# Attention and two MLPs in one kernel: groups of turned blocks without empty columns, an earlier request for auxiliary rows, a weight split in 16 pieces, x halves and sums in other places

## What is computed

```python
# 4 batches, 8 heads each (32 heads), 576 positions, head size 64
scores = q @ k.T / 8
cum = cumsum(max(s, 0))
scores = where(causal, -1e9, scores + min(-(cum_i - cum_j), 0))
attn = softmax(scores);  x = attn @ v            # tokens 2304, width 512
h = x @ w_in                                     # 512 -> 1024
solu = h * softmax(h);  x2 = layernorm(solu) * g_ln @ w_out   # 1024 -> 512
out = max(x2 @ w1, x2 @ w2, x2 @ w3) @ w_out2    # 512 -> 768 -> 512
```

## Time and profile before

| | |
|---|---|
| runs | 734.2, 733.35, 732.66 us; median 733.35 |
| the profiled execution | 731.73 us, its span 729.9 us |
| granted TensorE clock | 0.999 of full speed |
| TensorE matmul | 704.8 us busy, 97% of the span |
| VectorE | 388.5 us, 53%; from 100 to 200 us: 95.0 us of 100 |
| ScalarE | 319.0 us, 44%; from 100 to 200 us: 89.3 us of 100 |
| GpSimd | 253.6 us, 35%; from 100 to 200 us: 86.6 us of 100 |
| DMA | 59.5 MB, 82 GB/s over the span; 160 to 220 GB/s in the attention stage |

### The profile page before, as it was taken

One profiled execution on the slowest core, in us unless ns is written; L12 is line 12 of the kernel. 1 busy time (PEld: TensorE's weight loads), 2 busy tenths in 40 slices (PEclk: granted clock), 3 DMA queues, 4 the chain that ended last, 5 costly groups with the idle time before them and its releaser, 6 DMA issues.

```text
span 729.9 us, 12004 instructions
## 1 busy us (share of the span) xinstructions
PE 704.8 (97%) x4032; PEld 621.7 (85%) x4032; DVE 388.5 (53%) x681; ACT 319.0 (44%) x752; POOL 253.6 (35%) x284
## 2 busy tenths in 40 slices
PE   3899999999999999999999999999999999999998
PEld 3798898888887898989898998888888888888897
DVE  7999999999968556363635445510320132022121
ACT  3899998899865335242424423311210121111111
POOL 8767778898889464343101000000000000000000
PEclk9999999999999999999999999999999999999999
DMA  6577777778476140900000031001000000100000
GB/s 185 169 205 228 190 199 190 190 195 227 124 175 145 46 87 11 250 0 1 1 1 1 0 116 58 0 1 58 0 1 30 29 1 1 57 1 0 30 30 30
DMA packets 57721, 59.52 MB, mean 82 GB/s; under 512 B 23060, under 2 KB 44692, under 8 KB 57652
## 3 DMA queue, kind: packets, MB, share of 16 engines
q1 hardware_dynamic: 57684, 59.02, 30.1%
HBM read 44.15 MB, written 10.10 MB: 74 GB/s over the span
## 4 chain that ended last, share of the span: by engine, by line
PE 77%; DVE 9%; issue 6%; ACT 5%; POOL 3%; DVEq 0%; ACTq 0%; POOLq 0%
PE ps L680 10%; PE ps L682 10%; PE ps L681 10%; PE ps L597 5%; PE ps L599 5%; PE ps L598 5%; PE ps L523 4%; PE ps L525 4%; PE ps L524 4%; PE ps L489 4%; PE ps L698 3%; PE ps L700 3%; PE ps L699 3%; DVE q_a L1063 3%; DVE nmax L1070 3%
## 5 line engine op out<-in xcount | busy, mean ns | idle before, releaser
L682 PE MATMUL ps<-x_lo,w_hi 128*128 128x512 f32 (+1 forms) x360 | 132.4, 368 | 0.0
L681 PE MATMUL ps<-x_hi,w_lo 128*128 128x512 f32 (+1 forms) x360 | 132.4, 368 | 0.0
L680 PE MATMUL ps<-x_hi,w_hi 128*128 128x512 f32 (+1 forms) x360 | 132.4, 368 | 0.0
L870 ACT ACTIVATE probs<-ps,nmax 128x576 f32<-128x576 f32 (+4 forms) x160 | 82.9, 538 | 6.7 <-DVE nmax L1070 6.7
L489 PE MATMUL ps<-ident,probs 128*128 128x128 f32 x480 | 75.8, 282 | 8.4 <-DVE pt_lo L1077 5.6
L1077 DVE TENSOR_TENSOR pt_lo<-ps,pt_hi 128x512 fp32r<-128x512 f32 (+1 forms) x128 | 78.3, 653 | 7.7 <-ACT pt_hi L880 4.8
L682 PEld LDWEIGHTS ps<-x_lo,w_hi 128*128 128x128 f32 x360 | 67.9, 189 | 11.3
L681 PEld LDWEIGHTS ps<-x_hi,w_lo 128*128 128x128 f32 x360 | 67.9, 189 | 11.2
L680 PEld LDWEIGHTS ps<-x_hi,w_hi 128*128 128x128 f32 x360 | 67.9, 189 | 11.2
L880 ACT ACTIVATE pt_hi<-ps 128x512 fp32r<-128x512 f32 (+1 forms) x128 | 69.8, 574 | 11.6 <-PE ps L489 9.3
L471 PE MATMUL ps<-k_a,q_a 128*128 128x288 f32 (+2 forms) x192 | 63.2, 336 | 11.4 <-POOL qk_b L743 10.8
(11 more groups left out here) (100 smaller groups left out, 1416.9 us busy)
## 6 DMA issues: line engine op xcount, KB each, us to landing
qk_raw<-in_qk_dram SPq DMA_DIRECT2D x32, 576.0 KB, 4.4
xT<-halves SPq DMA_DIRECT2D x32, 144.0 KB, 2.4
xb_dram<-halves SPq DMA_DIRECT2D x32, 144.0 KB, 2.4
xb<-xb_dram SPq DMA_DIRECT2D x24, 192.0 KB, 3.7
rinvB<-rsum_dram SPq DMA_DIRECT2D x24, 192.0 KB, 4.7
stage<-in_moe_w_dram SPq DMA_DIRECT2D x18, 256.0 KB, 4.6
out_dram<-stage SPq DMA_DIRECT2D x18, 256.0 KB, 2.0
v_raw<-in_v_dram SPq DMA_DIRECT2D x32, 128.0 KB, 3.7
```

The source lines that it names most:

```text
L680: pe.matmul(dst, w_hi[f][:, i, c, :], x2_hi[par][:, c, 0:w], start=(c == 0), stop=False)
L681: pe.matmul(dst, w_lo[f][:, i, c, :], x2_hi[par][:, c, 0:w], start=False, stop=False)
L682: mm = pe.matmul(dst, w_hi[f][:, i, c, :], x2_lo[:, c, CT * g:CT * g + w], start=False, stop=(c == KC - 1))
L870: act.activation(dst, SCORES[c], ACT.Exp, bias=nmax[par][:, c:c + 1], accum_out=sums_all[:, c, bass.ds(t, 1)]).then_inc(exp_done, 1)
```

## The change

It has five parts. The groups of turned blocks are put together anew and the area of `pt_hi` and `pt_lo` is laid out to match, and group 0 leaves out the 64 empty columns of block (0, 0). SP requests the auxiliary rows of head t-1 before it waits for and requests q and k of head t. `w_in` is split in 16 pieces of 256 columns, one after each slot from slot 12 to 27. In the first MLP's group 0 the x halves for the next group come before the exponential on ScalarE, and on VectorE right after the maximum, with `wout_low` in their old place. VectorE inverts the sums of heads 0 to 23 after slot 26.

```diff
-    J2, J0, J1, J4, J3, TW = 0, 3 * P, 8 * P, 12 * P, 13 * P, 15 * P
+    J0, J2, J1, J4, J3, TW = 0, 5 * P, 8 * P, 12 * P, 13 * P, 15 * P
     GROUPS = [
-        ([(2, 2), (2, 3), (2, 4), (0, 0)], J2),
-        ([(0, 1), (0, 2), (0, 3), (0, 4)], J0 + P),
+        ([(0, 0), (0, 1), (0, 2), (0, 3)], J0),
+        ([(0, 4), (2, 2), (2, 3), (2, 4)], J0 + 4 * P),
...
-        WPIECES = 8
+        WPIECES = 16
         WPIECE = KC * FF // WPIECES
+        WFIRST = HEADS // 2 - 2 - WPIECES // 2
...
             def reload(t, par, known=None):
+                if known == 3:
+                    sp.wait_ge(aux_stored, 16)
+                if known is None or known >= 3:
+                    reload_aux(t - 1, 1 - par)
                 sp.wait_ge(k_hi_ready, t - 1)
                 sp.wait_ge(q_lo_ready, t - 1)
                 sp.wait_ge(k_lo_ready, t - 1)
                 load_qk(t, par)
                 if known is None or known >= 4:
                     reload_v(t - 2, par)
-                if known == 3:
-                    sp.wait_ge(aux_stored, 16)
-                if known is None or known >= 3:
-                    reload_aux(t - 1, 1 - par)
...
-            FIRST = HEADS // 2 - 1 - WPIECES
-            with pool.Fori(2, FIRST) as pair:
+            with pool.Fori(2, WFIRST) as pair:
...
-            with pool.Fori(FIRST, HEADS // 2 - 1) as pair:
+            with pool.Fori(WFIRST, WFIRST + WPIECES // 2) as pair:
                 t = 2 * pair
                 slot(t, 0, None)
+                split_win(t - 2 * WFIRST)
                 slot(t + 1, 1, None)
-                split_win(pair - FIRST)
+                split_win(t + 1 - 2 * WFIRST)
+            for t in range(2 * WFIRST + WPIECES, HEADS - 2):
+                slot(t, t % 2, t)
...
-                n = P * len(blocks)
-                act.activation(pt_hi[1 - par][:, o:o + n], ps[:, GBANK[g], 0:n], ACT.Copy).then_inc(pt_hi_done, 1)
+                skip, n = PAD if g == 0 else 0, P * len(blocks)
+                act.activation(pt_hi[1 - par][:, o + skip:o + n], ps[:, GBANK[g], skip:n], ACT.Copy).then_inc(pt_hi_done, 1)
...
                     ab = (base + i) % 2
+                    if first and i > 0:
+                        x_high(g + 1, i - 1, ab, False)
                     if not (first and i == 0):
                         gate(g, i, ab, first)
                     if i == 0 and not first:
                         x_high(g, 2, ab, first)
-                    elif i > 0 and more:
+                    elif i > 0 and more and not first:
                         x_high(g + 1, i - 1, ab, False)
...
-                n = P * len(blocks)
-                dve.tensor_tensor(pt_lo[1 - par][:, o:o + n], ps[:, GBANK[g], 0:n], f32(pt_hi[1 - par][:, o:o + n]),
-                                  ALU.subtract).then_inc(pt_lo_done, 1)
+                skip, n = PAD if g == 0 else 0, P * len(blocks)
+                dve.tensor_tensor(pt_lo[1 - par][:, o + skip:o + n], ps[:, GBANK[g], skip:n],
+                                  f32(pt_hi[1 - par][:, o + skip:o + n]), ALU.subtract).then_inc(pt_lo_done, 1)
...
-            with dve.Fori(2, HEADS // 2 - 2) as pair:
+            with dve.Fori(2, HEADS // 2 - 3) as pair:
                 t = 2 * pair
                 slot(t, 0, None)
                 slot(t + 1, 1, None)
-            invert_sums(1, slice(0, LAST))
-            for t in range(HEADS - 4, HEADS):
+            for t in range(HEADS - 6, HEADS):
                 slot(t, t % 2, t)
+                if t == HEADS - 6:
+                    invert_sums(1, slice(0, LAST))
...
                 if first and i > 0:
-                    wout_low(range(i + 2, i + 3))
+                    x_low(g + 1, i - 1, ab)
...
                     if i == 0:
                         x_low(g, 2, ab)
-                    elif i > 0 and more:
+                    elif first:
+                        wout_low(range(i + 2, i + 3))
+                    elif more:
                         x_low(g + 1, i - 1, ab)
```

## The result

The changed kernel takes 728.83 us (median of 5 runs, 728.23 to 729.56) against 733.35 (5 runs). The ratio is 0.9949, 95% interval 0.9938 to 0.996: 2.9 to 4.5 us faster, where 2.0 was forecast. The profiled execution spans 726.4 us against 729.9.

What follows compares the result with a forecast made beforehand. TensorE, 97% busy, was taken as the bound, with attention stalls made by GpSimd. Terms -0.9 + 0.5 - 1.8 + 0 + 0.2 = -2.0 us took the profiled 731.73 to 729.7, forecast as 731.3 for the median; range 727.5 to 734.9.

Steps and rivals of the forecast that it cites:

- C: w_in in 16 pieces of 256 columns, one per slot from slot 12: GpSimd's cycle 6.14 us, -1.8 us.
- B: Auxiliary rows requested ahead of q and k: their delay mostly absorbed, +0.5 us (bounds 0 and +2.2).
- E: Sums inverted after slot 26: VectorE's 1.65 us moved ahead of slot 27's q_low, +0.2 us (bounds -0.9 and +1.0).
- A: Group 0 without empty columns, 448 wide: 0.07 us in some 16 slots GpSimd does not set, -0.9 us.
- D: x halves ahead of the exponential in MLP group 0: 0.5 us of idle time only moves, 0.
- the second: GpSimd's slots become the bound, kernel slower; pieces of 1.89 us give +3.9, 737.3 us; chance 0.13.
- the third: q and k of heads 8, 10, 12 land later by all of 0.68 us: sum -0.3, 733.1 us; chance 0.20.
- The first: GpSimd keeps pace in the attention slots, cycle 5.64 us under 5.91: sum -5.6, 727.8 us; chance 0.20.

Runs made afterwards that it cites:

- experiment 3: The kernel before with w_in split in 16 pieces from slot 12 alone: 729.33 us, ratio 0.9955.
- experiment 1: The kernel before with the new groups and without the 64 empty columns alone: 731.27 us, ratio 0.9978.
- experiment 5: The changed kernel with the old groups and the 64 empty columns back: 729.64 us, ratio 0.9965 to the kernel before.
- experiment 11: The changed kernel with the 256 KB weight requests moved right behind q and k of the odd head: 728.5 us, ratio 0.9936 to the kernel before.
- Experiment 8: The changed kernel with each piece's high part made by tensor_scalar and the loop written out: 727.07 us, ratio 0.9926 to the kernel before.
- B alone: The kernel before with the auxiliary rows requested ahead of q and k alone: 731.6 us, ratio 0.9982.
- experiment 6: The changed kernel with the inversion of the sums back in front of slot 28: 729.73 us, ratio 0.9956 to the kernel before.
- experiment 4: The kernel before with the inversion of the sums after slot 26 alone: 733.25 us, ratio 0.9999.

## Why the prediction was right, and which term was mis-sized

The sign and the range held, and so did the mechanism of the largest term: GpSimd's cycle sets the slots with pieces. The other terms were less well founded. The sum said -2.0; the ratio says -3.7 (-2.9 to -4.5).

**C was the term that was too small**: -1.8 forecast, -3.3 alone (-2.3 to -4.2), -2.85 in its profile (109.96 in place of 112.81 over slots 13 to 30). The rates were right: a piece of 1.47 for 1.5, a cycle of 6.12 for 6.14, a slot 0.20 over the undisturbed one for 0.23. The first half of the working was right too, that the old pieces cost 4.9: experiment 3 leaves 1.18 us over the pitch in slot 27, and 1.1 had been set aside for the waits of B and E. The step that failed is the cost of the new pieces, "12 x 0.23, with 0.3 of recovery", 3.1 us. Ten slots lost 2.0 and nothing came behind, 2.1 in all with 0.1 in slots 13 to 16: slot 16 was still free, and in slot 27 GpSimd's lateness lay under the waits that were there anyway.

**A**: -0.9, from 0.07 us in the 16 slots that GpSimd does not set. Alone -1.6. The step that failed is where it pays: undisturbed slots did not change (experiment 1), and the gain lay in the slots beside the pieces of 512 columns, which the prediction left out. With the smaller pieces it was worth 0.2 us in the profiles (experiment 5) and 0.8 by the medians, with intervals that overlap. Why 64 columns gave 1.6 us beside the large pieces, more than 0.07 a slot, stays open.

**B**: +0.5 was too careful. The term that failed is the delay of q and k, which cost nothing: slots 4 to 12 take 54.69 us with the rows first and 54.73 without. GpSimd took heads 8, 10 and 12 0.27 us after landing in both, and by the times of the profiles they landed 0.35 and 1.6 us later and 1.3 us earlier with the rows first; a shift of 0.68 can't be told in that. That the weights before them hold these transfers up, experiment 11 shows by taking the weights away. B is 0 in the joined kernel as far as the runs can tell.

**D**: 0, and by the way foretold: the stop moved to `ln`, where 0.53 became 1.64.

**E**: +0.2 forecast; nothing alone by the runs, with 1.1 us more in its two slots. In the joined kernel the runs do not tell it from nothing, and the profiles show none: slots 27 to 30 take 25.06 us with it and 25.09 in experiment 3 without it. What I had not seen: the addition's time depends on what GpSimd does beside it (0.22 to 1.51).

Of the rivals, the second (a piece above 1.67) did not happen, and of the third (q and k later) nothing shows in the slots. The first was wrong for the changed kernel, since the cycle stayed above the slot's. Experiment 8 reaches the slots that it names, 5.93 us, by a lighter piece.

The parts alone add up to -1.6 - 1.3 - 3.3 + 0 = -6.2, and together they give -3.7. A and C overlap, as experiments 1 and 5 show by their profiles (1.6 us alone, 0.2 beside the new pieces); the runs of B alone say more than its profile, and what of that is scatter stays open. That the sum of the prediction came within 2 us owes something to luck: C was short by 1.0, and by the profiles of the joined kernels A (-0.2 for -0.9) and B (0 for +0.5) were off in opposite directions.

## What to carry to other kernels

When several engines are nearly full, time each one's own cycle from head to head and compare it with the slot. Here the one whose cycle was the slot's was GpSimd, though VectorE was busier: 0.29 us less work on GpSimd gave 0.18 a slot, and 0.07 less on VectorE gave nothing. Work that comes in lumps beside such a cycle is better spread evenly, and a stall that another engine causes anyway is a place to hide a part of it. A large transfer requested just ahead of one that is needed soon can hold it up: here q and k landed 0.9 to 2.4 us later behind 256 KB of weights. And a single profile of a kernel like this can differ from the next by 1.7 us in a stretch where nothing was changed, so a gain is read from the stretch where the change lies.

## What was not expected of the hardware

VectorE's addition over 128x120 elements, with a single input from SBUF, took 0.39, 0.71 and 1.51 us in three kernels, and 0.22 in experiment 6, where GpSimd stood idle beside it:

```profile
180.63 0.22 DVE L1090 TENSOR_SCALAR sums_all<-sums_all 128x120 f32<-128x120 f32 x1
```

In experiment 4 it started at 176.15 with this row of GpSimd's order of time:

```profile
176.15 1.41 POOL L743 TENSOR_TENSOR qk_b<-qk_raw,k_a 64x576 fp32r<-64x576 f32 x1
```

and ended at 177.66, 0.10 us after it. The Trainium skill (SBUF — State Buffer, "Who interferes with whom") says that `tensor_scalar` can enter a mode that uses the port shared with GpSimd, and that the other then waits for the whole instruction; this row agrees. `k_low` of GpSimd takes 1.92 us in place of 1.41 when `q_low` has started 0.20 before it, so the hold goes either way by the order of start, as that section says.

By the durations of its matmuls the higher TensorE clock came during slot 1 in 6 of 14 profiles and before its beginning in the others, with the same work until then. It makes 1.4 us in slot 1, of which 0.6 to 1.1 are left at slot 4.
